# First-batch scratch traffic of an FFT and MoE kernel: from DRAM round trips to SBUF-to-SBUF transfers

## The reference

```python
X = np.fft.rfft(x, axis=1)                    # x: (4, 3008, 256)
Y = X * (filt_r + 1j * filt_i)[None, :, :]
y = np.fft.irfft(Y, n=3008, axis=1)
h = np.maximum(y @ w_in, 0.0)                 # 256 -> 2048
z = (h * h) @ w_out                           # 2048 -> 256
g = z @ w_gate; val = z @ w_val               # 256 -> 1536
out = (g * sigmoid(g) * val) @ moe2_w_out     # 1536 -> 256
```

## Time and profile before

| | us |
|---|---|
| runs of the kernel before | 2362.91, 2357.90, 2362.17 (median 2362.17) |
| the profiled execution's own time | 2358.64 |
| its span in the profile | 2356.8 |
| TensorE busy | 2329.5 (99%) |
| VectorE, ScalarE busy | 1601.1 (68%), 1272.7 (54%) |
| granted TensorE clock, mean | 0.997 |
| first matmul of the feed-forward layer | 84.37 after the start |

### The profile page before, as it was taken

One profiled execution on the slowest core, in us unless ns is written; L12 is line 12 of the kernel. 1 busy time (PEld: TensorE's weight loads), 2 busy tenths in 40 slices (PEclk: granted clock), 3 DMA queues, 4 the chain that ended last, 5 costly groups with the idle time before them and its releaser, 6 DMA issues.

```text
span 2356.8 us, 31292 instructions
## 1 busy us (share of the span) xinstructions
PE 2329.5 (99%) x10581; PEld 1903.6 (81%) x10581; DVE 1601.1 (68%) x2707; ACT 1272.7 (54%) x2468; POOL 61.2 (3%) x124
## 2 busy tenths in 40 slices
PE   8899999999999999999999999999999999999999
PEld 4688888888888888888888878888888888888887
DVE  3567766677666776566555777777777777777776
ACT  4566656566655665555544445555555555555554
POOL 0100000000000000000000000000000000000000
PEclk9899999999999999999999999999999999999999
DMA  9643433333333333101002101001011011010000
GB/s 270 207 132 96 129 96 107 91 107 112 101 98 99 99 106 122 29 27 42 27 19 72 50 1 36 23 14 36 1 36 36 1 36 36 1 36 28 10 19 18
DMA packets 95423, 153.74 MB, mean 65 GB/s; under 512 B 10080, under 2 KB 48416, under 8 KB 94976
## 3 DMA queue, kind: packets, MB, share of 16 engines
q1 hardware_dynamic: 82112, 132.96, 17.9%
q0 software_dynamic: 13152, 18.78, 3.3%
HBM read 101.89 MB, written 49.81 MB: 64 GB/s over the span
## 4 chain that ended last, share of the span: by engine, by line
PE 96%; DMA 2%; SPq 1%; ACT 1%; issue 1%; DVE 1%; POOL 0%; ACTq 0%; DVEq 0%
PE psum L1450 31%; PE psum L1452 31%; PE psum L1451 31%; PE psum L1552 1%; DMA filt0b<-filt 1%; PE psum L1554 1%; PE psum L1461 1%; DMA B_scratch<-b_out 0%; SPq L562 0%; SPq L557 0%; PE psum L1504 0%; DMA w<-w_full 0%; ACT turned L820 0%; DMA A_scratch<-a_out 0%; ACT z_raw L820 0%
## 5 line engine op out<-in xcount | busy, mean ns | idle before, releaser
L1217 DVE SCALAR_TENSOR_TENSOR prod<-psum,act_out 128x512 f32<-128x512 f32 (+1 forms) x384 | 260.9, 679 | 398.4 <-ACT act_out L917 397.9
L917 ACT ACTIVATE act_out<-psum 128x512 f32<-128x512 f32 (+1 forms) x384 | 226.1, 589 | 461.5 <-PE psum L1452 461.2
L1450 PE MATMUL psum<-g_hi,m_hi 128*128 128x512 f32 (+1 forms) x768 | 305.7, 398 | 2.0 <-ACT z_raw L820 1.8
L1450 PE MATMUL psum<-v_hi,m_hi 128*128 128x512 f32 (+1 forms) x768 | 297.7, 388 | 1.5 <-DVE v_lo L1115 1.5
L1452 PE MATMUL psum<-v_hi,m_lo 128*128 128x512 f32 (+1 forms) x768 | 296.7, 386 | 0.0
L1451 PE MATMUL psum<-v_lo,m_hi 128*128 128x512 f32 (+1 forms) x768 | 296.7, 386 | 0.0
L1452 PE MATMUL psum<-g_hi,m_lo 128*128 128x512 f32 (+1 forms) x768 | 296.5, 386 | 0.0
L1451 PE MATMUL psum<-g_lo,m_hi 128*128 128x512 f32 (+1 forms) x768 | 296.4, 386 | 0.0
L1115 DVE TENSOR_TENSOR g_lo<-prod,g_hi 128x512 fp32r<-128x512 f32 (+1 forms) x408 | 270.6, 663 | 1.1 <-ACT g_hi L820 1.0
L820 ACT ACTIVATE g_hi<-prod 128x512 fp32r<-128x512 f32 (+1 forms) x408 | 248.5, 609 | 0.9 <-DVE prod L1251 0.9
L1450 PE MATMUL psum<-g_hi,m_out 128*128 128x512 f32 (+1 forms) x576 | 226.0, 392 | 0.3 <-DVE g_lo L1115 0.3
(11 more groups left out here) (125 smaller groups left out, 4246.9 us busy)
## 6 DMA issues: line engine op xcount, KB each, us to landing
filt_in<-filt SPq DMA_DIRECT2D x36, 512.0 KB, 3.9
z_scratch<-z_raw SPq DMA_DIRECT2D x23, 512.0 KB, 2.9
b_in<-B_scratch SPq DMA_DIRECT2D x122, 96.0 KB, 2.8
zq_raw<-z_scratch SPq DMA_DIRECT2D x44, 256.0 KB, 3.5
B_scratch<-b_out SPq DMA_DIRECT2D x38, 256.0 KB, 2.1
A_scratch<-a_out SPq DMA_DIRECT2D x50, 192.0 KB, 2.1
x_in<-x SPq DMA_DIRECT2D x48, 192.0 KB, 2.8
a_in<-A_scratch SPq DMA_DIRECT2D x36, 256.0 KB, 3.3
```

The source lines that it names most:

```text
L917: nc.scalar.activation(act_out[n % 2][:, 0:w], psum[:, n % 3, 0:w], ACT.Relu).then_inc(relu_done, 1)
L1217: nc.vector.scalar_tensor_tensor(out=prod[n % 2][:, 0:w], in0=psum[:, n % 3, 0:w], scalar=0.0, in1=act_out[n % 2][:, 0:w], op0=ALU.max, op ...
L1450: nc.tensor.matmul(dst, wh, vh, start=start, stop=False, skip_group_check=True)
```

## The change

For batch 0, A goes from `a0_out` to `a0` by 24 DMAs from SBUF to SBUF, one for each k2, each from 4 partitions of 32 KB to 128 partitions of 1 KB. They wait for all 16 copies of A, and they are issued behind all six filter transfers, which now follow `w23_0` directly. B goes for its first 6 blocks from `b0_out` to `b0_in` by 24 DMAs from SBUF to SBUF, two for each pair, each from 24 partitions to 4 partitions of 6 KB; the rows of the inverse matrix are permuted so that these blocks lie in the first 24 partitions. The other 26 blocks are stored to DRAM by GpSimd, for all 12 pairs. ScalarE's copy into a buffer of B waits for its moves also. All eight transfers of feed-forward weights are issued by SP between the moves of the first five pairs of B. `keep_busy` is issued 5 and 4 times in place of 9 and 7. `x0` and `a0_out` change places in SBUF.

```diff
-    w23_full = np.concatenate([fwd, swapped, inv, turn], 1)
+    rows = np.arange(P).reshape(P // NP, NP)
+    first = np.concatenate([rows[:, 0:PAIR * G0].reshape(-1), rows[:, PAIR * G0:].reshape(-1)])
+    w23_full = np.concatenate([fwd, swapped, inv[:, first], turn], 1)
...
+    R = P // NP
+    HERE, REST = PAIR * G0, NP - PAIR * G0
+    B0_d = nc.dram_tensor("B0_scratch", [UPS, R * REST, PAIR, D], F32, kind="Internal").ap()
...
-            def store_a0(n):
-            def load_a0(n):
+            def move_a0(n):
+                sp.wait_ge(a0_copied, PGS)
+                for k in range(K_CUTS[n], K_CUTS[n + 1]):
+                    sp.dma_start(a0[:, k, :], a0_out[R * k:R * (k + 1), :, :]).then_inc(a0_loaded[n], 16)
...
-            def store_last_b0(u):
-            def load_b0(n):
-            def load_last_b0():
+            def move_b0(u):
                 sp.wait_ge(b0_copied, u + 1)
                 for k in range(PAIR):
+                    rows = slice(PAIR * R * u + k, PAIR * R * (u + 1), PAIR)
+                    sp.dma_start(b0_in[rows, :, :], b0_out[u % 4][0:R * HERE, k, :]).then_inc(b0_moved[u % 4], 16)
...
             sp.dma_start(w23_0[:, :], w23_full).then_inc(w23_0_loaded, 16)
-            for n in range(len(A_CUTS) - 1):
-                store_a0(n)
-            load_filter0(0)
-            for n in range(3):
-                load_a0(n)
-            for n in range(1, len(FILT_CUTS) - 1):
+            for n in range(len(FILT_CUTS) - 1):
                 load_filter0(n)
-                if n + 2 < len(K_CUTS) - 1:
-                    load_a0(n + 2)
+            for n in range(len(K_CUTS) - 1):
+                move_a0(n)
             sp.dma_start(w4_0[:, :, :, :], w4_full).then_inc(w4_0_loaded, 16)
-            load_w_in(0)
-            load_w_out(0)
-            for n in range(UPS // 2 - 2):
-                load_b0(n)
-            store_last_b0(UPS - 2)
-            load_b0(UPS // 2 - 2)
-            store_last_b0(UPS - 1)
-            load_last_b0()
-            sp.wait_ge(b0_last_loaded, 16 * PAIR)
-            for k in range(1, 4):
-                load_w_in(k)
-                load_w_out(k)
+            for u in range(UPS):
+                move_b0(u)
+                if u < 4:
+                    load_w_in(u)
+                    load_w_out(u)
...
-                pool.dma_start(B_d[0, u], b0_out[u % 4][:, :, :]).then_inc(b0_stored[u % 4], 16)
+                pool.dma_start(B0_d[u], b0_out[u % 4][R * HERE:, :, :]).then_inc(b0_stored[u % 4], 16)
...
                 if u >= 4:
                     act.wait_ge(b0_stored[u % 4], 16 * (u // 4))
+                    act.wait_ge(b0_moved[u % 4], 16 * PAIR * (u // 4))
...
-            keep_busy(9)
+            keep_busy(5)
...
-            keep_busy(7)
+            keep_busy(4)
```

More of the change, by code:

```diff
@@ L134, in build @@
     A_d = nc.dram_tensor("A_scratch", [B, K2, P, D], F32, kind="Internal").ap()
-    B_d = nc.dram_tensor("B_scratch", [B, UPS, P, PAIR, D], F32, kind="Internal").ap()
+    R = P // NP
+    HERE, REST = PAIR * G0, NP - PAIR * G0
+    B0_d = nc.dram_tensor("B0_scratch", [UPS, R * REST, PAIR, D], F32, kind="Internal").ap()
+    B_d = nc.dram_tensor("B_scratch", [B - 1, UPS, P, PAIR, D], F32, kind="Internal").ap()
     z_d = nc.dram_tensor("z_scratch", [TILES, P, CH, T], F32, kind="Internal").ap()
@@ L214, in build @@
         W_IN = CH * F1 // PIECE
[L215 to L218, removed]
+        a0_out, at = place(0, "a0_out", [ROWS, NP, D])
+        assert at <= m1_lo_at
+        x0, at = place(m1_lo_at, "x0", [QP, NP, D])
+        assert at <= m1_end
         a0, at = place(g_region, "a0", [P, K2, D])
@@ L281, in build @@
         CUTS = [0, 1, 2, 4, 6, 8, 10, 12, 14, 16]
-        A_CUTS = [0, 4, 8, 12, 14, 15, 16]
         K_CUTS = [0, 2, 4, 8, 12, 16, 20, 24]
@@ L300, in build @@
         a0_copied = sem("a0_copied")
-        a0_stored = sem("a0_stored")
         a0_loaded = [sem(f"a0_loaded{n}") for n in range(len(K_CUTS) - 1)]
@@ L308, in build @@
         b0_stored = [sem(f"b0_stored{k}") for k in range(4)]
-        b0_loaded = sem("b0_loaded")
-        b0_last_stored = [sem(f"b0_last_stored{k}") for k in range(2)]
-        b0_last_loaded = sem("b0_last_loaded")
+        b0_moved = [sem(f"b0_moved{k}") for k in range(4)]
         s4_0_done = sem("s4_0_done")
@@ L477, in a0_pair @@
         def a0_pair(j):
-            half, i = divmod(j, PGS // 2)
-            return a0_out[half][:, PAIR * i:PAIR * (i + 1), :]
+            return a0_out[:, PAIR * j:PAIR * (j + 1), :]
         def as_f32(tile_ap):
@@ L486, in flat, with b_rows @@
             return tile_ap.rearrange("p a b -> p (a b)")
-        def b_rows(b, k):
-            return B_d[b, :, :, k, :].rearrange("u (r p) d -> (u r) p d", p=NP)
+        def b_rows(b, k, lo, hi):
+            if b == 0:
+                return B0_d[:, :, k, :].rearrange("u (r p) d -> (u r) p d", p=REST)[:, lo - HERE:hi - HERE, :]
+            return B_d[b - 1, :, :, k, :].rearrange("u (r p) d -> (u r) p d", p=NP)[:, lo:hi, :]
         def w_in_count(k):
@@ L615, in store_b @@
                 sp.wait_ge(b_copied, u + 1)
-                sp.dma_start(B_d[b + 1, k], b_out[u % 2][:, :, :])\
+                sp.dma_start(B_d[b, k], b_out[u % 2][:, :, :])\
                   .then_inc(b_stored[u % 2], 16)
@@ L623, in load_b @@
                     for h in range(4):
-                        sp.wait_ge(b0_stored[h], 16 * -(-(UPS - 2 - h) // 4))
-                    for h in range(2):
-                        sp.wait_ge(b0_last_stored[h], 16)
+                        sp.wait_ge(b0_stored[h], 16 * UPS // 4)
                 elif i == 0:
@@ L631, in load_b @@
                 for k in range(PAIR):
-                    sp.dma_start(b_in[g % 2][k:ROWS:PAIR, :, :], b_rows(b, k)[:, PAIR * i:PAIR * (i + 1), :])\
+                    sp.dma_start(b_in[g % 2][k:ROWS:PAIR, :, :], b_rows(b, k, PAIR * i, PAIR * (i + 1)))\
                       .then_inc(b_loaded[g % 2], 16)
@@ L803, in load_w4 @@
                 pool.dma_start(w4[g % 2][:, :, :, :], w4_table[g % PGS, :, :, :, :]).then_inc(w4_loaded[g % 2], 16)
-            for u in range(UPS - 2):
+            for u in range(UPS):
                 store_b0(u)
@@ L1477, in s2_0 @@
                 if PAIR * u in K_CUTS:
-                    pe.wait_ge(a0_loaded[K_CUTS.index(PAIR * u)], 16)
+                    n = K_CUTS.index(PAIR * u)
+                    pe.wait_ge(a0_loaded[n], 16 * (K_CUTS[n + 1] - K_CUTS[n]))
                 wait(pe, m0_done, u - 1)
@@ L1498, in s4_0 @@
                     pe.wait_ge(b0_copied, UPS)
-                    pe.wait_ge(b0_loaded, 16 * (UPS - 2))
-                    pe.wait_ge(b0_last_loaded, 16 * PAIR)
+                    for h in range(4):
+                        pe.wait_ge(b0_moved[h], 16 * PAIR * UPS // 4)
                 for n in range(PAIR * G0):
```

10 lines of the change are left out of this document (removed).

## The result

| | before | after |
|---|---|---|
| median of the runs, us | 2360.03 (4 runs) | 2393.43 (4 runs, 2392.40 to 2395.12) |
| profiled execution, us | 2358.64 | 2393.52 |
| span, us | 2356.8 | 2391.6 |
| mean granted clock | 0.997 | 0.988 |
| stage 4 of batch 0 starts at | 77.45 | 111.18 |

The ratio is 1.0142, with a 95% interval of 1.0125 to 1.016: slower by 33.4 us. The profiled executions differ by 34.9, and 32.7 of that is there when the feed-forward layer starts (117.04 - 84.37). The time went into the run-up of batch 0.

A forecast was written before the change was run, and what follows sets the result against it. TensorE was busy 2329.5 of 2356.8 us, the rest sought in batch 0's run-up, where the exchanges cost 8.4 and 11.0. Stage 4 moving from 77.45 to 105.9 added 28.4 to 2358.64: 2387.0, range 2361 to 2460.

The forecast's parts named there:

- the likeliest case: Exchange of A: four engines at 1.25 to 2.3 us a move, queue behind it, 2370 to 2396 us; chance 0.50.
- The second exchange by itself: From B's last copy to stage 4 of batch 0: 3.4 us in place of 11.0, a gain of 7.6.
- When the first exchange starts: First moves of A begin only at 36.4, behind all filters, though A is ready at 23.9.
- How fast it goes: Moves of A: four engines at 16.9 GB/s each, 1.94 us a move, 46.6 us for 24, complete at 83.0.
- What is queued behind it: Fifth copy of B waits past 83.0, ninth until 98.4; stage 4 at 105.9 in place of 77.45, +28.4 us.
- The clock: Around stage 4 of batch 0: no gain counted; possibly up to 5 us less, or up to 2 more.
- all 16 engines share: Rival on the moves: all 16 engines serve them, stage 4 at 73.7 (-3.8), about 2355 us; chance 0.17.
- The four source partitions bound the move: Rival on A's moves: the partitions read set 3.7 us a move, stage 4 at 148.5, +71, 2430 us; chance 0.28.
- The wait for the moves of B doesn't bite: Rival: B's moves overtake or weights don't delay them; stage 4 at 93, +16, 2374 us; no separate chance.

## Why the prediction held, and where it was off

The forecast was +28.4 us, 2387.0; the profiled execution shows +34.9, and the likeliest case was the right one: four engines, a slow first exchange, and a queue behind it that holds back the moves of B. By its steps:

- *The second exchange by itself* was to become a tail of 3.4 us. It is 6.7: from the end of the last copy, 104.44, to 111.18. **This is the term that was mis-sized most**, by 3.3. I priced two moves at what two loads had cost on quiet engines, and in the changed kernel the stores and tables that GpSimd issues and SP's first loads of x and B move beside them, at a share of 1.44 at 110. Where those were held back and GpSimd issued the moves, it took 3.2 us from the first of the last two issues to stage 4 (73.08 to 76.28), near the 3.36, and where only SP's weights came later, on SP's queue, the tail was still 6.0. So the traffic beside the moves or the queue makes the difference; the two aren't separated.
- *When the first exchange starts*: 36.4 was predicted, about 33.6 measured, since the filters kept 199 to 208 GB/s and not 190. It is 2.8 early.
- *How fast it goes*: four engines, shown by the closing packets and by the share of a quarter on one queue and on two. A move takes 2.00 us and not 1.94; 24 of them 48 us, to about 82 where I had 83.0. That this number came out so well is partly luck. I took 16.9 GB/s for an engine from loads out of DRAM and held it fixed; on the same quarter of the engines the runs show 25 GB/s in all for a lone move, 54 beside stores of B, 77 in a quiet stretch, and 94 from two queues, and 2.00 us is the mean of such stretches.
- *What is queued behind it*: the fifth copy waits until 83.87, behind all of A. The ninth came at 99.3 (98.4 predicted), and the end of the twelfth 5.1 us later and not 4.1, because TensorE did the stage 3 work between them at the lower clock (3.77 us for four records).
- *The clock*: I counted no gain, with up to 5 less at most. Stage 4 began at full clock and lost it: 4.37 against 5.42 us, 1.05 less. The first steps gave this back, with a granted clock of 0.76 at 127 to 132 where the kernel before, at the same distance from its first feed-forward matmul (94 to 99), had 1.00; from 117.04 on the kernel loses another 2.1 us.

The sum for stage 4 is -2.8 + 1.7 + 2.0 + 1.0 + 3.3 = +5.2 on 105.9, which is the 111.18 measured (the terms are start, moves, wait to the ninth copy, copies to the twelfth, tail). So 5.3 of the 6.5 us between forecast and measurement are there when stage 4 starts; the other 1.2 are the 1.05 less in stage 4, the 2.1 behind it and 0.1 outside the span. The term at the start was off in the other direction, which made the total look better than its terms.

Of the rivals, *all 16 engines share* falls with the share of 0.26, and the run from GpSimd shows what it would have been worth and what not: A keeps pace with TensorE, and the kernel is still 12.9 us slower than before, not the 3.7 faster that I gave this case (3.8 was the shift of stage 4). The wait of copies for buffers, the late filters and the tail remain. *The four source partitions bound the move* has its price wrong, 3.7 us a move against 2.00, but not all of its mechanism: a lone move went at 25 GB/s from neighbouring partitions, and partitions 32 apart gave 48 from the start. In the kernel, with moves overlapping, what part of the 2.00 us is due to them is open. (Its 148.5 comes to 148.1 from 3.7 us a move; nothing hangs on it.) *The wait for the moves of B doesn't bite* falls with the fifth copy, whose buffer came 15.1 us late.

One thing the prediction took for granted and did not question: that an earlier start of stage 4 is worth its length. The runs say otherwise. A stage 4 that starts 7 us earlier (weights last) gave 1.1, and more filler ahead of it gave nothing, as long as the loads of the first steps stood behind the weights.

## What to carry to other kernels

Before a DRAM round trip is replaced by SBUF to SBUF transfers, count the rows of the outermost dimension: a move out of 4 partitions ran on 4 of 16 DMA engines on both hardware queues, and put the exchange at 54 to 77 GB/s, where the stores of A through DRAM had run at 434. Transfers from 16 partitions to 16 kept 95% of the engines busy and ran at 142, but no kernel with such moves was tried. Moves out of few partitions block the queue behind them, so look at which buffer is released by the last transfer in that queue. And a gain ahead of a stage must be followed into the stage behind it: here it went in part to the next loads and to the clock behind the wait for them.

## What was not expected

- The same move from 4 partitions runs at 25 GB/s alone, at 48 in a row of eight and at 77 in the kernel, with the same quarter of the engines busy. From partitions 32 apart it starts at 43 to 50 in place of 25.
- From GpSimd's queue the same moves keep all 16 engines busy, with many small packets (1197 of 1575), at 157 GB/s in the kernel and 82 in the kernel that only times them.
- A transfer of 512 KB put between such moves cost 4.4 us of the queue, where 512 KB at the filters' 208 GB/s are 2.5.
- More `keep_busy` ahead of stage 4 gained nothing in the total until the loads of the first steps were issued ahead of the weights; together they held stage 4 at 2.4 GHz, 2.5 us shorter, and gave 2.3 us. That kernel, at 2356.19, keeps both exchanges in DRAM.
